# A fused attention and two-stage MLP kernel: softmax closed within its selection step, and two places for an expert tile's token parts

## The reference

```python
scores = q @ k.T / sqrt(64)              # batch 4, 8 heads, 576 positions, head size 64
kth = the 32nd largest of each row
attn = exp(where(scores >= kth, scores, -1e9) - max); attn /= sum + 1e-9
x = attn @ v                             # as 2304 tokens x 512
h = x @ w_in                             # 512 x 2048
x = (relu(h) + log1p(exp(-abs(h)))) @ w_out
logits = x @ w_gate                      # 8 experts, each token goes to its best
out = p_best * (relu(x @ w1[e]) @ w2[e]) # 512 -> 1024 -> 512, e = argmax(logits)
```

## Time and profile before

| what | value |
| --- | --- |
| median of 3 runs | 1056.23 us (1055.35 to 1056.42) |
| profiled execution | 1057.04 us, of it the span of the profile 1054.8 us |
| TensorE busy | 992.9 us (94%) |
| TensorE weight loads busy | 806.3 us (76%) |
| VectorE busy | 817.3 us (77%) |
| ScalarE busy | 727.6 us (69%) |
| GpSimd busy | 711.9 us (67%) |

### The profile page before, as it was taken

One profiled execution on the slowest core, in us unless ns is written; L12 is line 12 of the kernel. 1 busy time (PEld: TensorE's weight loads), 2 busy tenths in 40 slices (PEclk: granted clock), 3 DMA queues, 4 the chain that ended last, 5 costly groups with the idle time before them and its releaser, 6 DMA issues.

```text
span 1054.8 us, 21596 instructions
## 1 busy us (share of the span) xinstructions
PE 992.9 (94%) x6878; PEld 806.3 (76%) x6879; DVE 817.3 (77%) x1744; ACT 727.6 (69%) x1390; POOL 711.9 (67%) x831
## 2 busy tenths in 40 slices
PE   5565899999999999999999999999999999999996
PEld 2343687788788788788788888887887788888875
DVE  7999999999999999999999999994345622222261
ACT  3888898988998998998888999998554111111140
POOL 2688898889899899899888899899351311111101
PEclk9996899999999999999999999999999999999999
DMA  9723253343344343324434333333481421111100
GB/s 311 257 91 127 112 171 121 128 143 121 114 153 165 114 157 121 124 98 144 169 119 155 117 120 102 121 121 121 156 331 54 165 96 52 40 40 40 40 20 20
DMA packets 43391, 130.99 MB, mean 124 GB/s; under 512 B 4320, under 2 KB 18656, under 8 KB 33056
## 3 DMA queue, kind: packets, MB, share of 16 engines
q1 hardware_dynamic: 40256, 120.09, 32.5%
q0 software_dynamic: 3040, 9.70, 2.7%
HBM read 111.95 MB, written 18.09 MB: 123 GB/s over the span
## 4 chain that ended last, share of the span: by engine, by line
PE 80%; DVE 8%; POOL 4%; ACT 3%; issue 3%; DMA 1%; SPq 1%; ACTq 0%; DVEq 0%; POOLq 0%
PE psum L614 8%; PE psum L575 7%; PE psum L644 7%; PE psum L737 6%; PE psum L739 6%; PE psum L738 6%; PE psum L646 6%; PE psum L645 6%; PE psum L663 6%; PE psum L665 6%; PE psum L664 6%; PE psum L589 5%; DVE top L1158 3%; DVE work L1164 3%; PE psum L769 2%
## 5 line engine op out<-in xcount | busy, mean ns | idle before, releaser
L1158 DVE MAX8 top<-work 128x8 f32<-128x576 f32 x432 | 305.4, 752 | 0.0
L1164 DVE MATCH_REPLACE8 work<-top,work 128x576 f32<-128x576 f32 x288 | 212.6, 749 | 0.0
L644 PE MATMUL psum<-x_parts,wi_hi 128*128 128x256 f32 x576 | 171.1, 297 | 0.0
L645 PE MATMUL psum<-x_parts,wi_hi 128*128 128x256 f32 x576 | 162.9, 283 | 0.0
L646 PE MATMUL psum<-x_parts,wi_lo 128*128 128x256 f32 x576 | 162.7, 283 | 0.0
L614 PE MATMUL psum<-prT,vtok 128*64 128x128 f32 (+3 forms) x1600 | 117.1, 287 | 15.2 <-ACT prT L918 15.2
L614 PEld LDWEIGHTS psum<-prT,vtok 128*64 128x64 f32 (+1 forms) x1600 | 85.5, 144 | 54.2 <-issue 41.2
L575 PE MATMUL psum<-kT,qT 64*128 64x512 f32 (+3 forms) x640 | 113.0, 480 | 11.5 <-DMA qT<-in_q 4.4
L1638 POOL DMA_INDIRECT out<-ys,dst_now x19 | 19.2, 1012 | 152.6 <-DVE ys L1360 150.7
L663 PE MATMUL psum<-wo_ring,h_hi 128*128 x288 | 119.1, 414 | 1.0 <-POOL h_lo L1547 0.9
L1541 POOL TENSOR_TENSOR hs<-hs,ab 128x512 f32<-128x512 f32 x72 | 93.7, 1301 | 32.7 <-ACT ab L941 32.5
(11 more groups left out here) (215 smaller groups left out, 2353.1 us busy)
## 6 DMA issues: line engine op xcount, KB each, us to landing
wo_ring<-wo_parts SPq DMA_DIRECT2D x72, 1024.0 KB, 4.8
wo_parts<-wo_ring SPq DMA_DIRECT2D x8, 1024.0 KB, 3.8
kT<-in_k SPq DMA_DIRECT2D x16, 288.0 KB, 3.4
qT<-in_q SPq DMA_DIRECT2D x16, 288.0 KB, 3.9
vtok<-in_v SPq DMA_DIRECT2D x16, 256.0 KB, 2.9
wo_raw<-in_moe_w_out SPq DMA_DIRECT2D x1, 4096.0 KB, 14.1
wi_raw<-in_moe_w_in SPq DMA_DIRECT2D x4, 1024.0 KB, 14.4
x_rows<-x2tok SPq DMA_DIRECT2D x16, 256.0 KB, 2.4
```

The source lines that it names most:

```text
L644: nc.tensor.matmul(ps[:, part, :], wi_hi[:, u, kk, f], hi, start=first, stop=False)
L645: nc.tensor.matmul(ps[:, part, :], wi_hi[:, u, kk, f], lo, start=False, stop=False)
L1158: nc.vector.max(top[:, at, 8 * r:8 * r + 8], sc_of(n)[:, t, :] if r == 0 else work[:, t, :]).then_inc(topk_step, 1)
L1164: nc.vector.match_replace(work[:, t, :], top[:, at, 8 * r - 8:8 * r], sc_of(n)[:, t, :] if r == 1 else work[:, t, :], TAKEN).then_inc(topk ...
```

## The change

The start and the steady steps:
- In steps below 10 ScalarE scales block i-1 at the end of step i (normalise(i-1)) instead of block i-2 at its head, with probs_out(i-2) first. TensorE turns block i-2 and multiplies it by V ahead of the scores. GpSimd makes all denominators; VectorE keeps the reciprocal alone, of block n-1, ahead of the last maxima of block n.
- From step 10 on ScalarE makes the exponentials of block i-2 at the head of step i, then x_out, scores_out, h_high, and then the scaling. The cut-off of block i-1 stands behind probs_out. GpSimd's order becomes biases, mask, softplus, x_split_up, denominators, h_low.
- The scores are made two blocks ahead and not three from step 10 on, and step 9 has none. Block 7 is copied and split in step 9. FREE is 9, so block 8 has two cut-offs.
- The two bias instructions become one, with a table of factors. w_out is loaded by two DMAs with a semaphore each.

The experts: xsT_hi and xsT_lo have two places, in turn, in what was a gap. turn_xs(1) stands inside the last down product. turn_h(0) and count_late stand inside e_up(1) at its fourth and sixth part, turn_h(1) and slots_late each one part later in e_down(0) than before. VectorE makes relu(1) ahead of in_slots.

Left out of the diff below are the declarations of semaphores and the lines that only pass the new argument on.

```diff
@@ -89,7 +89,7 @@
-    FREE = MLP_AT - 2
+    FREE = MLP_AT - 1
...
@@ -209,9 +210,8 @@
         sb("gap_d", [P, WLEN])
-        xsT_hi = sb("xsT_hi", [P, KD, P], F32R)
-        xsT_lo = sb("xsT_lo", [P, KD, P], F32R)
-        sb("gap_x", [P, 2 * KD * P])
+        xsT_hi = sb("xsT_hi", [P, 2, KD, P], F32R)
+        xsT_lo = sb("xsT_lo", [P, 2, KD, P], F32R)
         xs = sb("xs", [P, XS, DM])
...
@@ -329,13 +331,17 @@
-        AHEAD = 3
+
+        RING = 5
...
         def scores_at(i):
-            return i + 1 if i <= 0 else i + AHEAD
+            return i + 1 if i <= 0 else i + 3 if i < MLP_AT - 1 else i + 2 if i >= MLP_AT else BLOCKS
+
+        def scores_made(i):
+            return min(i + 4, MLP_AT + 2) if i < MLP_AT else min(i + 3, BLOCKS)
...
@@ -453,7 +459,10 @@
                 load_v(0, p)
-            sp.dma_start(wo_raw[:], w_out.rearrange("(k p) n -> p k n", p=P)).then_inc(wo_loaded, 16)
+            for half in range(2):
+                at = slice(half * KF // 2, (half + 1) * KF // 2)
+                sp.dma_start(wo_raw[:, at, :], w_out.rearrange("(k p) n -> p k n", p=P)[:, at, :]
+                             ).then_inc(wo_loaded[half], 16)
             for kk in range(KD):
...
@@ -577,11 +586,11 @@
-            def turn_probs(n):
+            def turn_probs(n, made):
                 if n:
...
                     pe.wait_ge(x_copied, n)
-                pe.wait_ge(scores_copied, 2 * min(scores_at(n + 2) + 1, BLOCKS))
+                pe.wait_ge(scores_copied, 2 * made)
                 for t in range(2):
...
@@ -797,16 +806,26 @@
                 n = scores_at(i)
+                if i < MLP_AT:
+                    if late:
+                        turn_probs(i - 2, scores_made(i - 1))
+                        times_v(i - 2)
+                    if is_block(n):
+                        scores(n, max(i - 1, 0))
+                    if i == 0:
+                        scores(n + 1, 0)
+                        scores(n + 2, 0)
+                    continue
...
                 if up_at(i) and up_at(i)[1] == 0 and is_block(n):
-                    amid[0, k_last(up_at(i)[0])] = lambda: scores(n, max(i - 2, 0))
+                    amid[0, k_last(up_at(i)[0])] = lambda: scores(n, i - 2)
                 elif is_block(n):
-                    scores(n, max(i - 2, 0))
+                    scores(n, i - 2)
                 if up_at(i):
...
                 if late:
-                    turn_probs(i - 2)
+                    turn_probs(i - 2, scores_made(i))
                 if i in TURNS:
...
@@ -816,9 +835,6 @@
                     times_v(i - 2)
-                if i == 0:
-                    scores(n + 1, 0)
-                    scores(n + 2, 0)
...
@@ -849,26 +865,26 @@
             last_down(6)
-            e_up(0, rank_first, halves=True, parts=(0,))
-            last_down(7)
-            e_up(0, rank_first, {(1, 1): lambda: turn_tokens(LASTG, NT - 2, 5),
-                                 (1, 2): lambda: turn_tokens(LASTG, NT - 1, 4),
-                                 (1, 3): lambda: logits(NT - 2, 3)}, halves=True, parts=(1,))
+            e_up(0, 0, rank_first, halves=True, parts=(0,))
+            down(LASTG, UNITS - 1, 0)
+            turn_xs(1, 1)
+            down(LASTG, UNITS - 1, 1)
+            e_up(0, 0, rank_first, {(1, 1): lambda: turn_tokens(LASTG, NT - 2, 5),
+                                    (1, 2): lambda: turn_tokens(LASTG, NT - 1, 4),
+                                    (1, 3): lambda: logits(NT - 2, 3)}, halves=True, parts=(1,))
             logits(NT - 1, 7)
-            turn_xs(1, 1)
-            turn_h(0)
-            e_up(1, rank_first, {(0, 1): count_late})
-            e_down(0, 0, rank_first, {KE // 2: lambda: turn_h(1), KE // 2 + 1: slots_late}, halves=True)
+            e_up(1, 1, rank_first, {(0, 3): lambda: turn_h(0), (1, 1): count_late})
+            e_down(0, 0, rank_first, {KE // 2 + 1: lambda: turn_h(1), KE - 2: slots_late}, halves=True)
             e_down(1, 1, rank_first, {KE - 2: lambda: turn_xs(2, 2)})
             pe.wait_ge(tiles_ready, 1)
-            e_up(2)
+            e_up(2, 0)
             turn_xs(3, 3)
...
                 with live(T + 1):
-                    e_up(T + 1)
+                    e_up(T + 1, (place + 1) % 2)
                 with live(T + 2):
...
@@ -949,7 +965,7 @@
             def split_wo(u):
-                act.wait_ge(wo_loaded, 16)
+                act.wait_ge(wo_loaded[u // (UNITS // 2)], 16)
                 if u >= 2:
...
@@ -1010,11 +1026,11 @@
-            def xs_out(T):
+            def xs_out(T, xpar):
                 act.wait_ge(xs_turned, T + 1)
-                if not (isinstance(T, int) and T == 0):
-                    act.wait_ge(e_h_raw, T)
-                nc.scalar.copy(xsT_hi[:].rearrange("p k t -> p (k t)"),
+                if not (isinstance(T, int) and T < 2):
+                    act.wait_ge(e_h_raw, T - 1)
+                nc.scalar.copy(xsT_hi[:, xpar].rearrange("p k t -> p (k t)"),
                                psum[:, 0, :]).then_inc(xs_copied, 1)
...
@@ -1038,52 +1054,58 @@
                     if late:
-                        normalise(i - 2, 0)
-                        normalise(i - 2, 1)
-                    if is_block(i - 3):
-                        x_out(i - 3)
+                        probs_out(i - 2)
                     if now:
...
                             cut_off(i - 1, t)
-                    scores_out(scores_at(i))
                     if wo_unit(i) is not None:
...
                         exponentials(i - 1, 0)
+                    if late and i == MLP_AT - 1:
+                        x_out(i - 2)
+                    if now:
                         exponentials(i - 1, 1)
-                    if late:
-                        probs_out(i - 2)
-                    if wi_unit(i) is not None:
-                        split_wi(wi_unit(i))
+                    if late and i < MLP_AT - 1:
+                        x_out(i - 2)
+                    if is_block(scores_at(i)):
+                        scores_out(scores_at(i))
                     if i == 0:
...
                         scores_out(scores_at(i) + 2)
+                    if now:
+                        normalise(i - 1, 0)
+                        normalise(i - 1, 1)
+                    if wi_unit(i) is not None:
+                        split_wi(wi_unit(i))
                     continue
+                behind = late and i > MLP_AT
+                if behind:
+                    exponentials(i - 2, 0)
+                    exponentials(i - 2, 1)
+                if is_block(i - 3) and i > MLP_AT:
+                    x_out(i - 3)
+                if is_block(scores_at(i)):
+                    scores_out(scores_at(i))
                 if up_at(i - 1):
                     h_high(*up_at(i - 1))
-                if is_block(i - 3):
-                    x_out(i - 3)
-                if now:
-                    for t in cuts(i - 1):
-                        cut_off(i - 1, t)
-                if is_block(scores_at(i)):
-                    scores_out(scores_at(i))
-                if late:
+                if behind:
                     normalise(i - 2, 0)
...
                     probs_out(i - 2)
+                if now:
+                    for t in cuts(i - 1):
+                        cut_off(i - 1, t)
                 if i in TURNS:
...
                     logarithm(*up_at(i))
-                if now:
-                    exponentials(i - 1, 0)
-                    exponentials(i - 1, 1)
                 if down_at(i) and down_at(i)[1] == UNITS - 1:
...
@@ -1112,23 +1134,23 @@
             logarithm(LASTG, 7)
-            xs_out(0)
+            xs_out(0, 0)
             h_high(LASTG, 7)
...
             first_w2(1)
+            xs_out(1, 1)
             down_out(LASTG)
...
             logits_out(NT - 2, 3)
+            e_relu_out(0)
             logits_out(NT - 1, 7)
...
-            e_relu_out(0)
-            xs_out(1)
             gate_exps(1)
...
             e_h_out(1, 1)
-            xs_out(2)
+            xs_out(2, 0)
             act.wait_ge(splits_ready, 1)
...
@@ -1165,13 +1187,10 @@
             def reciprocals(n):
-                if n < MLP_AT - 1:
-                    dve.wait_ge(exp_ready, 2 * n + 2)
-                    nc.vector.tensor_reduce(den[:, n % 2, :], eps[:, n % 2], AX.X, ALU.add
-                                            ).then_inc(den_step, 1)
                 dve.wait_ge(den_step, n + 1)
+                if n >= 2:
+                    dve.wait_ge(pr_ready, 2 * n - 2)
                 nc.vector.reciprocal(rden[:, n % 2, :], den[:, n % 2, :]).then_inc(rden_ready, 1)
...
@@ -1183,13 +1202,10 @@
                             strike(n, t, r)
-                    if r == 1 and n > MLP_AT:
-                        reciprocals(n - 2)
+                    if r == ROUNDS - 1 and n:
+                        reciprocals(n - 1)
                     for t in range(2):
                         maxima(n, t, r)
```

(59 more changed lines are left out.)

30 lines of the change are left out of this document (17 added, 13 removed).

## The result

The changed kernel takes 1065.97 us, median of 4 runs (1065.75 to 1066.71), against 1056.33 us (1055.35 to 1058.16) for the kernel before beside it: ratio 1.0094, 95% interval 1.0080 to 1.0107. It is slower by 9.6 us. The forecast was 1062.0 us; the time lies inside the range, 4.0 us above the value. The profiled execution has a span of 1064.1 us, before 1054.8. All times in this document are of the chip's fast state; one run of the first kernel of experiment 9 (1179.12 us, mean granted clock 0.79) fell in the slower one and is left out.

What follows compares the result with a forecast made beforehand. VectorE was taken to bound the start, TensorE the rest, VectorE 2% behind. -2.1 (start and join) +3.6 +1.5 +2.3 +0.5 = +5.8 on 1056.23: 1062.0 us; likeliest case 1058 to 1066, 8 in 10 within 1053.5 to 1067.5.

Steps and rivals of the forecast that it cites:

- the ring and its 10.5 us: Start: chain from one block's scaling through turning, cut-off, subtractions, w_out's low part and reciprocal; 10.5 us slow, 9.8 fast.
- one of 10.2, two of 9.8: Start: after four periods of 10.5 us between scalings, the last three shorten; eighth scaling at 97.8.
- the first term: Join: turn_probs(8) waits for block 12's scores' copy, behind block 8's scaling and the last w_in split; some 1.5 us.
- some 2 us: Join, step 10: w_in's last low part (2.37 us) on GpSimd stands ahead of block 10's biases, now gating step 12.
- +3.6 forecast: Seven group borders: the h_high cast ahead of the scaling adds 0.51 us each while TensorE waits; +3.6 us.
- The term "+1.5": Plain steps and the one after a border: 0.2 us per step over seven groups, +1.5 us (ends 0 and 3).
- The ring through GpSimd: Plain steps: h_low, biases, masks, last exponential, x_out, scores_out and cast take 9.5 to 9.65 us against a 9.45 step.
- +2.3 forecast: End of attention: one more step with scores (1.2 us) and later steps coupled to VectorE; together +2.3 us.
- 3 x 0.36: End of attention, steps 70 to 73 without scores: they take VectorE's 9.70 us instead of 9.34.
- +0.5 forecast: Experts: late counts some 0.8 later, 0.80 relu wait won back; +0.5 us, 0 to +2, upper end at half rate.
- A start at VectorE's pace: Rival, chance 0.2: all seven start periods 9.72 us with fast turning, nothing handed back at the join; -2.4, 1053.8 us.
- the bound of the steady steps: Rival, chance 0.18: VectorE becomes the bound, 9.70 against 9.45, +5 in place of 1.5, slow start and experts; 1068 us.

Runs made afterwards that it cites:

- first kernel of experiment 9: Changed kernel with four repairs: denominators ahead of w_out's low part, border cast ahead of scores' copy, earlier w_in splits, first hidden low part ahead of late counts; 1053.83 us.
- first kernel of experiment 6: Changed kernel with the low part of the first expert tile's hidden values made by VectorE ahead of the late counts' chain; 1061.08 us.
- Experiment 3: Changed kernel with start-stage denominators ahead of w_out's low part, plus six unread identity transposes on TensorE behind each start step's scores; 1061.4 us.
- experiment 2: Changed kernel with GpSimd's denominators ahead of the low part of w_out in the start; 1065.23 us.
- experiment 5: Changed kernel with w_in's splits one step earlier from the fifth unit on, two of them in step 5; 1062.55 us.
- experiment 4: Changed kernel with the cast of the high part ahead of the scores' copy in the seven steps where a group begins; 1061.28 us.
- experiment 7: Changed kernel with ten unread identity transposes on TensorE between the second expert tile's up product and the first down product; 1063.99 us.
- experiment 8: Changed kernel with w_out in one load instead of two; 1068.5 us.
- experiment 1: Parts apart: attention alone, the changed kernel with the old expert order and one place for token parts, 1061.57 us; experts alone, kernel before with that part, 1059.46 us.

## Why the prediction was right in sign and 4 us short

**Start.** Right: the first reciprocal (25.68; forecast 25.7), the first scaling, the ring and its 10.5 us. What missed in the profiled execution is "one of 10.2, two of 9.8, as the turning speeds up late in this stage": all seven are slow, 0.9 us more by the eighth scaling. (The terms as written add up to 97.7, not 97.8.) The forecast of the mixture can't be called wrong by this trace alone: in others with the same start the eighth scaling stood at 97.30 to 98.95, though in none with the two fast periods at its end. By the rule of the Trainium skill (TensorE: Matmul & The Clock Gate, Part 1: The HAM clock gate) the prediction worked out seven periods of 10.5; the durations of the changed kernel agree with that, those of the first kernel of experiment 6 (periods of 10.49 and 9.70 side by side) do not. Experiment 3 shows that the level matters to the ring, and experiment 2 that GpSimd's low part was not alone in it.

**Join.** Right: that most is handed back, and by whom. Of the first term, 1.5 us for the wait of turning 8 for the scores' copy, 1.1 came: 0.4 is that wait (0.49 against 0.12), the rest mostly up(0,0), of which more ran at the slow clock than before. The size of the second, "some 2 us" for the last low part of w_in, was for the work alone, and this is the step that was mis-sized most. Step 12 took 4.0 us more than in the kernel before, and experiment 5 won 4.05 by taking the work away. The trace of experiment 6's first kernel splits it: with the same wait and no fall of the clock in it the step took 2.4 us more (11.82 against 9.46), so 2.4 is the late biases and the rest, some 1.6, the slower products behind TensorE's wait, as far as one trace of each tells. I had priced the wait and not what follows from it. The miss of 2.9 us at step 12 is 0.9 of the start, 0.2 up to up(0,0), and 1.8 from there.

**Borders.** +3.6 forecast, +3.6 measured, and 3.77 back in experiment 4.

**Plain steps.** The term "+1.5" was mis-sized. The scaling stands at t+3.08, as worked out, and that was enough: three plain steps took 9.41, 9.42 and 9.51 us, before 9.44, 9.45 and 9.45. Apart from the borders, the stretch from step 12 to 68 is 0.1 us longer. The ring through GpSimd that I had at 9.5 to 9.65 shows at most in the third plain step of a group (9.50 to 9.55), and the two ahead of it give that back: the lower end (0) of the range given.

**End of attention.** +2.3 forecast, 2.54 measured (steps 68 to 73: 47.20 us, before 44.66). Half of it is as worked out: step 69, which now has scores, is 1.25 longer (forecast 1.2). The other half is right in size only. "3 x 0.36" took 9.34 for each step before and 9.70 after; steps 70 to 73 took 9.09, 8.59, 9.35 and 9.01 before and 9.63, 8.79, 9.70 and 9.20 after, so one of them alone is at VectorE's 9.70. That 1.3 us came of it, near the 1.1 forecast, is luck. No run tried this stage by itself.

**Experts.** +0.5 forecast, +2.3 measured, over the upper end of 2. "Some 0.8 later" for the counts was 1.4, and, as at the join, the wait of 2.78 us brought a lower clock with it, worth 1.5. I had named half rate for those products as the upper end of the range and not taken it. From the late counts to the first w2 product it is 5.5 us, forecast 5.8, with TensorE idle ahead of it, as forecast. The kernel before had a fall of its own near here that cost it about 1 us.

The sum of the errors: start and join +2.9, rings -1.4, end +0.2, experts +1.8, makes 3.5; the remainder of 0.5 is between spans and medians. That the rings cost nothing hid 1.4 us of what the join and the experts had too small: with that term as forecast the time would have been over the 1066 us at which I ended the likeliest case.

**Rivals.** A start at VectorE's pace needs TensorE at its fast level, as its condition said; experiment 3 got 9.8 us periods that way, and the join kept the gain. But the rival also had the join hand nothing back, 33.9 us from the eighth scaling to times V of step 12 (130.3 less 1.4 and 95); experiment 3 took 38.5, and only with w_in's low part out of the way did it come to that (34.4 in experiment 5, 33.7 in the first kernel of 9). VectorE never became the bound of the steady steps: with all repairs they run at 9.99 us in the mean (step 13 to 68), as before (9.98).

## What to carry to other kernels

When a term of the sum is "TensorE waits n us", ask what slower products behind the wait would cost: at the first expert tile 2.78 us of waiting cost another 1.5, at the join 2.11 another 1.6, and in another execution a wait of 2.04 at the same place cost nothing more. When work is moved into an order by hand, write down every ring that the moved step closes, on each engine, and at the slow clock too: with one ring shortened another of the same length was right behind it. And put what heads a chain (the biases, the late counts, the scaling) ahead of bulk work in its queue: the repairs here are such swaps, and together they turned 9.6 us lost into 2.6 us won. Before a difference of 1 us between two single traces is put down to an edit, look at how far the traces of kernels differ ahead of the edit: in the start stage here it was up to 1.6 us.

## What the runs showed of the hardware

TensorE's granted clock fell to 0.50 right behind a wait of 2.11 us (at 132.40) and of 2.78 us (at 824.58) in stretches where it had stood at 1.00, and was back at 1.00 after some 5 us; with 1.78 us of wait left it fell as well (experiment 7). The length of the wait doesn't decide it: behind 2.04 us in experiment 6 (131.93), 2.01 in experiment 8 (136.45) and 1.57 in experiment 1 (attention alone, 133.38) it stayed at 1.00, and in the kernel before it fell at about 808 us with no wait over 0.42 us in the 20 us ahead. Waits of 0.55 us at borders left it at 1.00. The Trainium skill (TensorE: Matmul & The Clock Gate, HAM oscillation — how this bites in real kernels) tells of such falls where TensorE waits between bursts of products, and the changed kernel's two agree; the waits it tells of, 3 to 5 us for a load, are longer than these.

The column of the granted clock can't be trusted by itself. In experiment 2 it reads 1.00 all through the start (and in the kernel before up to 70 us, with eight transposes of 1.94 us at 63.85):

```profile
65.00:70.00 5.00, 2.90 (x12) 1.00 0.04 18
70.00:75.00 5.00, 3.79 (x27) 1.00 0.46 192
```

(windows of TensorE, columns as above), while eight transposes take 1.94 us and times V 2.60 (69.18 and 72.54 above), just as where it reads 0.50 in the changed kernel. The durations decide.
